# Two feed-forward blocks' up projections at a time, with the last 64 input rows as pairs of 64-row matmuls

## What is computed

```python
w = softmax(weight)                      # per head, over 7 taps
x = causal_conv(x, w)                    # 16384 tokens x 192
h = np.maximum(x @ moe_w_in, 0.0)        # 16384 x 2048
x = (h * h) @ moe_w_out                  # 16384 x 192
h = x @ moe2_w_in
g = np.where(h > 0.0, h, np.exp(np.minimum(h, 0.0)) - 1.0)
return g @ moe2_w_out
```

## Time and profile before

| | |
|---|---|
| time, median of 3 runs | 2363.64 us (2362.62 to 2364.51) |
| span of the profiled execution | 2362.3 us |
| mean granted TensorE clock | 0.998 |
| PE busy | 2328.2 us, 10240 matmuls |
| PEld busy | 1925.1 us, 10240 loads |
| DVE busy | 1693.1 us |
| ACT busy | 1520.5 us |
| POOL busy | 57.0 us |
| HBM read, written | 25.44 MB, 12.58 MB |

### The profile page before, as it was taken

How to read it: one execution, slowest core, us unless ns; L and a number is a source line. 1 busy time by engine, 2 the same in 40 slices (tenths; PEclk the granted TensorE clock), 3 DMA queues, 4 the chain that set the end, 5 groups by cost and what they waited for, 6 DMA issues and landing times.

```text
span 2362.3 us, 33660 instructions
## 1 busy us (share of the span) xinstructions
PE 2328.2 (99%) x10240; PEld 1925.1 (81%) x10240; DVE 1693.1 (72%) x2807; ACT 1520.5 (64%) x2766; POOL 57.0 (2%) x48
## 2 busy tenths in 40 slices
PE   5999999999999999999999999999999999999999
PEld 3888888888888888888888888888888888888887
DVE  7767777677776677776777767776667777677777
ACT  4766666666666666666666666666666666666664
POOL 6200000000000000000000000000000000000000
PEclk9999999999999999999999999999999999999999
DMA  4000000000000000000000000000000000000000
GB/s 143 19 8 16 9 16 16 9 14 14 12 16 16 7 16 9 16 16 7 16 9 16 16 16 7 16 9 16 16 7 16 9 16 16 7 16 14 12 7 14
DMA packets 66477, 38.19 MB, mean 16 GB/s; under 512 B 1952, under 2 KB 64416, under 8 KB 66464
## 3 DMA queue, kind: packets, MB, share of 16 engines
q1 hardware_dynamic: 66464, 38.03, 5.6%
HBM read 25.44 MB, written 12.58 MB: 16 GB/s over the span
## 4 chain that ended last, share of the span: by engine, by line
PE 97%; DVE 1%; DMA 0%; issue 0%; ACT 0%; SPq 0%; DVEq 0%
PE bank_a L286 10%; PE bank_b L287 10%; PE bank_a L283 10%; PE bank_a L282 10%; PE bank_b L284 10%; PE bank_h L265 10%; PE bank_h L263 10%; PE bank_h L266 10%; PE bank_h L264 10%; PE bank_h L262 10%; DVE conv_b L448 0%; DVE conv_a L448 0%; DVE act_lo L487 0%; DMA raw_down<-in_moe_w_out_dram 0%; DMA x_cols<-in_x_dram 0%
## 5 line engine op out<-in xcount | busy, mean ns | idle before, releaser
L487 DVE TENSOR_TENSOR act_lo<-act,act_hi 128x512 fp32r<-128x512 f32 x1024 | 712.7, 696 | 451.6 <-ACT act L353 448.7
L358 ACT ACTIVATE expo<-bank_h 128x512 f32<-128x512 f32 x512 | 306.5, 599 | 509.6 <-PE bank_h L266 506.3
L342 ACT ACTIVATE relu<-bank_h 128x512 f32<-128x512 f32 x512 | 306.4, 598 | 278.8 <-PE bank_h L266 273.5
L262 PE MATMUL bank_h<-mov_hi_a,up_hi_a 128*128 128x512 f32 x1024 | 399.1, 390 | 20.2 <-DVE mov_lo_b L453 20.2
L286 PE MATMUL bank_a<-act_lo,down 128*128 128x512 f32 x1024 | 399.5, 390 | 9.1 <-DVE act_lo L487 9.0
L263 PE MATMUL bank_h<-mov_lo_a,up_hi_a 128*128 128x512 f32 x1024 | 399.3, 390 | 0.0
L264 PE MATMUL bank_h<-mov_hi_a,up_lo_a 128*128 128x512 f32 x1024 | 399.1, 390 | 0.0
L266 PE MATMUL bank_h<-mov_lo_b,up_b 128*128 128x512 f32 x1024 | 399.1, 390 | 0.0
L265 PE MATMUL bank_h<-mov_hi_b,up_b 128*128 128x512 f32 x1024 | 399.1, 390 | 0.0
L284 PE MATMUL bank_b<-act_hi,down 128*128 128x512 f32 x1024 | 398.8, 389 | 0.0
L282 PE MATMUL bank_a<-act_hi,down 128*128 128x512 f32 x1024 | 398.8, 389 | 0.0
(11 more groups left out here) (45 smaller groups left out, 1861.0 us busy)
## 6 DMA issues: line engine op xcount, KB each, us to landing
x_cols<-in_x_dram SPq DMA_DIRECT2D x32, 536.0 KB, 4.3
out_dram<-res_a SPq DMA_DIRECT2D x32, 256.0 KB, 2.6
raw_up<-in_moe_w_in_dram SPq DMA_DIRECT2D x8, 512.0 KB, 6.3
out_dram<-out_b SPq DMA_DIRECT2D x32, 128.0 KB, 2.3
raw_down<-in_moe_w_out_dram SPq DMA_DIRECT2D x8, 384.0 KB, 7.0
x_cols<-in_x_dram SPq DMA_DIRECT2D x1, 512.0 KB, 4.1
taps<-in_weight_dram SPq DMA_DIRECT2D x1, 7.0 KB, 1.7
```

The source lines that it names most:

```text
L262: pe.matmul(bank, hi, hi_a, start=True, stop=False)
L487: dve.tensor_tensor(act_lo[s][:, :], act32[s][:, :], act_hi[s][:, :].bitcast(F32), ALU.subtract)\
```

## The change

The up projections of two neighbouring blocks are issued together by `up_pair`: for each block the three full matmuls on the first 128 channels, and then for the last 64 channels three pairs of 64-row matmuls, high x high, high x low and low x high. In a pair the even block uses partitions 0 to 63 and the odd block 64 to 127, each writing its own `bank_h`. So a pair of blocks has 12 up matmuls where two blocks had 10, and low x low of the last 64 channels is no longer computed. `up_b` is replaced by `up_hi_b` and `up_lo_b` of half its width, and the loads put even blocks' rows in the upper and odd blocks' rows in the lower partitions, in two DMAs. PE's order is now up_pair(j + 2), down_project(j), down_project(j + 1). The programs of ACT and DVE change only where weights are split.

```diff
             def load_chunk(c, w_in, w_out, loaded):
                 cols = slice(c * CF * P, (c + 1) * CF * P)
-                sp.dma_start(raw_up[:, :, cols], w_in[:, :, cols]).then_inc(loaded, 16)
+                sp.dma_start(raw_up[:, cols], w_in[:, 0, cols]).then_inc(loaded, 16)
+                pairs = slice(c * CF * DB, (c + 1) * CF * DB)
+                for odd, rows in ((0, slice(0, DB)), (1, slice(DB, P))):
+                    tiles = w_in[rows, 1, cols].rearrange("p (q two c) -> p q two c", two=2, c=P)
+                    sp.dma_start(raw_up_b[rows, pairs].rearrange("p (q c) -> p q c", c=P), tiles[:, :, odd, :])\
+                      .then_inc(loaded, 16)
...
-                pool.tensor_tensor(up_b[m][DB:P, cols], raw_up[DB:P, 1, cols],
-                                   up_b[m][DB:P, cols].bitcast(F32), ALU.subtract).then_inc(up_done, 1)
+                pool.tensor_tensor(up_lo_b[m][:, pairs], raw_up_b[:, pairs],
+                                   up_hi_b[m][:, pairs].bitcast(F32), ALU.subtract).then_inc(up_done, 1)
...
-            def up(b, kind, j):
+            def up_pair(b, kind, j):
...
-                bank = bank_h[j % HBANKS][:, :]
-                cols = slice(f * P, (f + 1) * P)
-                hi, lo, both = up_hi_a[m][:, cols], up_lo_a[m][:, cols], up_b[m][:, cols]
-                hi_a, lo_a, hi_b, lo_b = (t[:, :] for t in mov[h])
-                pe.matmul(bank, hi, hi_a, start=True, stop=False)
-                pe.matmul(bank, hi, lo_a, start=False, stop=False)
-                pe.matmul(bank, lo, hi_a, start=False, stop=False)
-                pe.matmul(bank, both, hi_b, start=False, stop=False)
-                pe.matmul(bank, both, lo_b, start=False, stop=True).then_inc(h_ready, 1)
+                hi_a, lo_a, hi_b, lo_b = mov[h]
+                for i in range(2):
+                    bank = bank_h[(j + i) % HBANKS][:, :]
+                    cols = slice((f + i) * P, (f + i + 1) * P)
+                    pe.matmul(bank, up_hi_a[m][:, cols], hi_a[:, :], start=True, stop=False)
+                    pe.matmul(bank, up_hi_a[m][:, cols], lo_a[:, :], start=False, stop=False)
+                    pe.matmul(bank, up_lo_a[m][:, cols], hi_a[:, :], start=False, stop=False)
+                pair = slice(f // 2 * P, (f // 2 + 1) * P)
+                for stationary, moving, stop in ((up_hi_b[m], hi_b, False), (up_hi_b[m], lo_b, False),
+                                                 (up_lo_b[m], hi_b, True)):
+                    for i, rows in ((0, slice(0, DB)), (1, slice(DB, P))):
+                        done = pe.matmul(bank_h[(j + i) % HBANKS][:, :], stationary[rows, pair], moving[rows, :],
+                                         start=False, stop=stop)
+                        if stop:
+                            done.then_inc(h_ready, 1)
...
-                for j in range(BLOCK):
-
-
-                    if j + AHEAD < BLOCK:
-                        up(b, kind, j + AHEAD)
+                for j in range(0, BLOCK, 2):
+                    if j + 2 < BLOCK:
+                        up_pair(b, kind, j + 2)
                     elif kind != END:
-                        if kind == FIRST and j + AHEAD == BLOCK:
+                        if kind == FIRST:
                             pe.wait_ge(w2_done, 4 * CHUNKS)
-                        up(b + 1, MIDDLE, j + AHEAD - BLOCK)
+                        up_pair(b + 1, MIDDLE, 0)
                     down_project(b, kind, j)
-
-            for j in range(AHEAD):
-                up(0, FIRST, j)
+                    down_project(b, kind, j + 1)
+
+            up_pair(0, FIRST, 0)
```

More of the change, by code:

```diff
@@ L47, in bass_conv_mlp_mlp_kernel @@
     LAST = TILES - 1
-    AHEAD = 3
     HBANKS = 4
@@ L52, in bass_conv_mlp_mlp_kernel @@
     CF = STEPS // CHUNKS
-    assert N == 512 and 2 * DB == P and STEPS % SLOTS == 0 and AHEAD == HBANKS - 1 and STEPS % HBANKS == 0
+    assert N == 512 and 2 * DB == P and STEPS % SLOTS == 0 and HBANKS == 4 and CF % 2 == 0 and STEPS % HBANKS == 0
     HI_A, HI_LO_B, LO_A = slice(0, P), slice(P, 2 * P), slice(2 * P, 3 * P)
@@ L73, in bass_conv_mlp_mlp_kernel @@
         up_lo_a = [sb(f"up{m}_lo_a", [P, FF], F32R) for m in (1, 2)]
-        up_b = [sb(f"up{m}_b", [P, FF], F32R) for m in (1, 2)]
+        up_hi_b = [sb(f"up{m}_hi_b", [P, FF // 2], F32R) for m in (1, 2)]
+        up_lo_b = [sb(f"up{m}_lo_b", [P, FF // 2], F32R) for m in (1, 2)]
         down = [sb(f"down{m}", [P, STEPS, 3 * P], F32R) for m in (1, 2)]
-        raw_up = sb("raw_up", [P, 2, FF])
+        raw_up = sb("raw_up", [P, FF])
+        raw_up_b = sb("raw_up_b", [P, FF // 2])
         raw_down = sb("raw_down", [P, STEPS, D])
@@ L222, in lo_parts @@
                 tiles = slice(c * CF, (c + 1) * CF)
-                pool.tensor_tensor(up_lo_a[m][:, cols], raw_up[:, 0, cols],
+                pairs = slice(c * CF * DB, (c + 1) * CF * DB)
+                pool.tensor_tensor(up_lo_a[m][:, cols], raw_up[:, cols],
                                    up_hi_a[m][:, cols].bitcast(F32), ALU.subtract).then_inc(up_done, 1)
                 pool.wait_ge(up_done, before + 1)
-                pool.tensor_tensor(up_b[m][DB:P, cols], raw_up[DB:P, 1, cols],
-                                   up_b[m][DB:P, cols].bitcast(F32), ALU.subtract).then_inc(up_done, 1)
+                pool.tensor_tensor(up_lo_b[m][:, pairs], raw_up_b[:, pairs],
+                                   up_hi_b[m][:, pairs].bitcast(F32), ALU.subtract).then_inc(up_done, 1)
                 pool.wait_ge(up_done, before + 2)
@@ L239, in _ @@
                 tiles = slice(c * CF, (c + 1) * CF)
-                pool.wait_ge(w2_loaded[c], 32)
-                pool.tensor_copy(up_hi_a[1][:, cols], raw_up[:, 0, cols]).then_inc(w2_hi_done, 1)
-                pool.tensor_copy(up_b[1][:, cols], raw_up[:, 1, cols]).then_inc(w2_hi_done, 1)
+                pool.wait_ge(w2_loaded[c], 64)
+                pairs = slice(c * CF * DB, (c + 1) * CF * DB)
+                pool.tensor_copy(up_hi_a[1][:, cols], raw_up[:, cols]).then_inc(w2_hi_done, 1)
+                pool.tensor_copy(up_hi_b[1][:, pairs], raw_up_b[:, pairs]).then_inc(w2_hi_done, 1)
                 pool.tensor_copy(down[1][:, tiles, 0:D], raw_down[:, tiles, :]).then_inc(w2_hi_done, 1)
@@ L314, in split_w1 @@
                 tiles = slice(c * CF, (c + 1) * CF)
-                act.wait_ge(w1_loaded[c], 32)
-                act.copy(up_hi_a[0][:, cols], raw_up[:, 0, cols]).then_inc(w1_hi_done, 1)
-                act.copy(up_b[0][:, cols], raw_up[:, 1, cols]).then_inc(w1_hi_done, 1)
+                act.wait_ge(w1_loaded[c], 64)
+                pairs = slice(c * CF * DB, (c + 1) * CF * DB)
+                act.copy(up_hi_a[0][:, cols], raw_up[:, cols]).then_inc(w1_hi_done, 1)
+                act.copy(up_hi_b[0][:, pairs], raw_up_b[:, pairs]).then_inc(w1_hi_done, 1)
                 act.copy(down[0][:, tiles, 0:D], raw_down[:, tiles, :]).then_inc(w1_hi_done, 1)
```

## The result

| | before | after |
|---|---|---|
| time, median | 2363.97 us (2362.62 to 2364.51, 4 runs) | 2696.42 us (2694.2 to 2697.14, 4 runs) |
| span of the profiled execution | 2362.3 us | 2692.3 us |

The ratio is 1.1406, with a 95% interval of 1.1392 to 1.142: the change costs 332 us.

The account below looks back on a forecast made before the run. PE was taken to bind the kernel, busy 99%. 224 coupled ELU pairs at 0.815 us and 217 ReLU pairs at 0.355 add 259.6 to 2363.6, giving 2623 us; the range was 2540 to 2810.

Parts of the forecast that it names:

- the coupling: Down projection of block j-1 waits on work behind block j on ACT and DVE: +0.705 us per ELU pair, +0.245 per ReLU.
- The likeliest case: Half rows side by side with a small entry price: 2560 to 2640 us, likeliest 2623; chance 0.51.
- the rival with a drain: PE drains at each switch of row size, 0.27 us each, the upper bound: 2714 us; chance 0.26.
- Half rows side by side, three slots a pair: On PE, six half-row matmuls take three slots of 0.2265 us, so a pair has 19 slots, not 20.
- The rival of one after another: The two halves of the array run in turn, 22 slots per pair: 2804 us; chance 0.14.
- The chain in the ELU half: From T, start of a pair's last half-row matmul, to the down projection's low matmul L286: 2.97 us, stalling PE 0.93.
- The price of the change of row size: PE going from full to half rows and back: 0.11 us at entry and at exit, between 0 and 0.27.
- The slot behind a restart: PE's spacing from one matmul to the next, taken as 0.2265 us throughout.
- Look-ahead enough: Rival: PE saves its slot and the down projection's low matmul never waits: 2248 us; chance 0.04.
- clock falls: Rival: PE's idle time lowers its clock, eight slots per coupled pair at the low level: about 3330 us; chance 0.03.
- Start and loads at nothing: Extra DMAs at the start and POOL's half-width low part: 0 us taken, with 5 us either way.

Follow-up runs that it names:

- d_same_half: Changed kernel with ACT and DVE finishing both blocks of a pair before the next, and both half-row matmuls on partitions 0 to 63: 2817.94 us, ratio 1.1921.
- f: Kernel before with the changed kernel's PE order, all rows full, and ACT and DVE finishing both blocks of a pair before the next: 2366.88 us, ratio 1.0013.
- a: Kernel before with the changed kernel's order on PE, all matmuls at full rows, ACT and DVE order unaltered: 2597.9 us, ratio 1.0991.
- c: Changed kernel with the three pairs of half-row matmuls moved ahead of the six full ones in each pair of blocks: 2535.22 us, ratio 1.0728.

## Why the prediction was right or wrong

The direction, the coupling and the range were right. The likeliest case was 73 us too low (2623 against 2696): the time lies outside the band of 2560 to 2640 that had most of the chance, and nearer to the rival with a drain (2714). The range held because it took that rival in, and not because the sum was good to the 20 us that were given for its latencies.

- **Half rows side by side, three slots a pair.** Right, in the changed kernel's timeline, and d_same_half shows that it hangs on the rows. The rival of one after another has no row for it.
- **The chain in the ELU half.** Forecast L286 at T + 2.97, measured T + 2.96; in the ReLU half T + 2.51 and 2.52 (1005.37 + 0.11 - 1002.96). The stalls come out smaller than the 0.93 and 0.47 us named: in the ReLU half 0.24 (1005.01 + 0.2265 to 1005.48), because the exit's 0.2 lies in it, as the prediction said it would; in the ELU half 0.58 (1041.13 to 1041.71), where the load of 0.10 behind the wait for the cast lies in it too.
- **The price of the change of row size.** This is the term that was mis-sized: 0.11 taken, 0.2 measured, at entry and at exit. The load ahead is lost, as I took it, but it also starts 0.09 later: at 1038.18, 0.32 after L272's start, where the slot would have begun 0.2265 after it. On 441 coupled pairs the entry's 0.09 is 40 us; on 63 uncoupled ones both are 11. I had chosen the nearest row, of a restart behind a wait; PE had stood idle there for longer than that, so the row could not show a delay of the load behind the matmul before it.
- **The slot behind a restart.** The prediction kept 0.2265 throughout; after an unhidden load a few slots are 0.23 to 0.24. With the 0.2 in place the pairs would be 5.435 and 4.975; they are 5.47 and 5.03, 224 x 0.035 + 217 x 0.055 = 20 us. Together 71 of the 73.
- **The Trainium skill's rule** (TensorEngine Tiling (Array Packing), Key Properties), that changing the tiling mode drains the TensorE, agrees with these rows: 0.09 us before the load can start. How far the array empties they don't show: the load starts 0.32 after L272 does, before the 0.39 of L272's row, whose end is modelled, is over. The upper bound I tied to it, 0.16 and 0.11, was more than the trace shows, so the sum by it was 18 us too high and not 73 too low; 0.26 was too small a chance for it.
- **Where the coupling comes from.** The prediction named two things together, the shorter distance between up and down and the order on ACT and DVE. The runs take them apart: the kernel before has this order with the longer distance and loses nothing, f has the shorter distance with the other order and loses nothing that can be told, a has both and loses 235 us. It takes both: the engines' order, unchanged, starts block j before it finishes j-1, and both blocks of a pair end together, with down(j-1) close behind. In c, where the even block ends three slots earlier, 161 us of the loss are gone.
- **Look-ahead enough, clock falls.** Neither. The granted clock was 1.00 for the whole execution, in the stretch of one tile too (columns as in rows 4):

```profile
1000.00:1083.00 83.00, 80.83 (x354) 52.95 (x352) 51.34 (x88) 46.61 (x88) 0.00 (x0) 1.00 0.04 11
```

- **Start and loads at nothing.** Right within what shows: PE's first matmul waits 19.9 us in place of 20.2, POOL's 49.9 busy us are off the path, and the last up matmul of the eighth pair starts at 64.9 in place of 67.8 us, 2.9 us earlier and inside the 5 us allowed either way.

## What to carry to other kernels

When the order of one engine is regrouped, look at the engines whose programs were written for the old order: here most of the loss, 227 of 332 us, was that ACT and DVE start a block before they finish the one before it, and a change of a few conditions took it away. Two half-row matmuls side by side take one slot, where from the same half they take two. But here three such pairs replaced four full matmuls, so each group saved one slot (0.2265 us), and going from full rows to half rows and back costs nearly two (0.41 us). Count entries and exits against saved slots before writing it, and take as the price a row in which the engine wasn't already idle. An engine's busy share hid all of this (96% against 99%), and the chain and the waits of the weight loads did not.

## What the runs showed that was not expected

The entry and the exit cost the same, 0.42 us from start to start against 0.2265, and half of the price above the slot (0.10) is the weight load that is no longer hidden. A group of half-row matmuls three or six pairs long has the same price, and so has one whose two matmuls don't run side by side (d: L277's load at 1034.28). Even with half as many changes the packing only breaks even here, at 9.07 against 9.06 us for four blocks.
